# Splitting the gated activations and dividing the attention rows on VectorE, out of a buffer in SBUF

## What is computed

```python
# attention: B, H, S, D = 2, 8, 768, 64; n_sink = 4, window = 128
scores = (q @ k.T) / sqrt(D)
keep = (pos_k < n_sink) | ((0 <= pos_q - pos_k) & (pos_q - pos_k < window))
a = softmax(where(keep, scores, -1e9))          # divided by (sum + 1e-9)
x = (a @ v), heads side by side                 # 1536 tokens x 512
# block 1: 512 -> 2048 -> 512
h = x @ w_in
x = (h * sigmoid(1.702 * h)) @ w_out
# block 2: 512 -> 1536 -> 512
out = (sigmoid(x @ w_gate) * (x @ w_val)) @ w_out2
```

## Time and profile before

| | |
|---|---|
| three executions | 715.40, 715.57, 716.10 us, median 715.57 us |
| the profiled one | 715.4 us, of which the span from first to last instruction is 713.6 us |
| mean granted clock of PE | 0.997 |
| opening stage | 0 to about 87 us |
| chunk 0, 1, 2 | to about 301.6, 521.9 and 711 us |

### The profile page before, as it was taken

How to read it: one execution, slowest core, us unless ns; L and a number is a source line. 1 busy time by engine, 2 the same in 40 slices (tenths; PEclk the granted TensorE clock), 3 DMA queues, 4 the chain that set the end, 5 groups by cost and what they waited for, 6 DMA issues and landing times.

```text
span 713.6 us, 10667 instructions
## 1 busy us (share of the span) xinstructions
PE 687.4 (96%) x3632; PEld 562.0 (79%) x3632; DVE 278.1 (39%) x820; ACT 397.4 (56%) x855; POOL 354.7 (50%) x419
## 2 busy tenths in 40 slices
PE   6777999999999999999999999999999999999998
PEld 5556788888788888788888788888878888788886
DVE  6888434344444333343443433333232222311112
ACT  4787466667665666466676666565444444433321
POOL 2574245555455545266565655464335445544530
PEclk9999999999999999999999999999999999999999
DMA  6322332343433223143325323311132233233001
GB/s 199 137 75 75 114 113 100 101 144 126 141 116 108 89 73 104 60 148 129 99 98 177 125 82 134 119 60 36 60 141 90 91 126 138 103 110 114 0 1 59
DMA packets 23798, 73.41 MB, mean 103 GB/s; under 512 B 3616, under 2 KB 3616, under 8 KB 23744
## 3 DMA queue, kind: packets, MB, share of 16 engines
q1 hardware_dynamic: 23744, 72.73, 30.9%
HBM read 69.57 MB, written 3.15 MB: 102 GB/s over the span
## 4 chain that ended last, share of the span: by engine, by line
PE 88%; ACT 4%; DVE 3%; issue 2%; SPq 1%; DMA 0%; ACTq 0%; DVEq 0%
PE ps L781 22%; PE ps L782 21%; PE ps L783 21%; PE ps L847 5%; PE ps L848 5%; PE ps L849 5%; PE ps L768 1%; PE ps L766 1%; PE ps L767 1%; PE ps L751 1%; PE ps L738 1%; PE ps L752 1%; PE ps L739 1%; ACT probs L434 1%; DVE probs_n L605 1%
## 5 line engine op out<-in xcount | busy, mean ns | idle before, releaser
L379 POOL TENSOR_TENSOR w_lo<-w_raw,w_hi 128x256 fp32r<-128x256 f32 (+1 forms) x336 | 277.4, 857 | 270.7 <-ACT w_hi L428 270.7
L781 PE MATMUL ps<-x_hi,w_hi 128*128 128x512 f32 x480 | 195.6, 407 | 1.2 <-issue 0.9
L782 PE MATMUL ps<-x_lo,w_hi 128*128 128x512 f32 x480 | 188.2, 392 | 0.0
L783 PE MATMUL ps<-x_hi,w_lo 128*128 128x512 f32 x480 | 187.6, 391 | 0.0
L428 ACT ACTIVATE w_hi<-w_raw 128x1024 fp32r<-128x1024 f32 (+1 forms) x84 | 104.3, 1242 | 42.5 <-PE ps L849 25.9
L621 DVE SCALAR_TENSOR_TENSOR ps<-squashed,ps 128x512 f32<-128x512 f32 x84 | 58.2, 692 | 151.2 <-PE ps L783 88.5
L452 ACT ACTIVATE g_hi<-ps 128x512 fp32r<-128x512 f32 x84 | 50.1, 597 | 110.9 <-DVE ps L621 110.9
L783 PEld LDWEIGHTS ps<-x_hi,w_lo 128*128 128x128 f32 x480 | 90.2, 188 | 20.0
L781 PEld LDWEIGHTS ps<-x_hi,w_hi 128*128 128x128 f32 x480 | 90.2, 188 | 15.8 <-issue 1.7
L782 PEld LDWEIGHTS ps<-x_lo,w_hi 128*128 128x128 f32 x480 | 90.6, 189 | 12.8
L626 DVE TENSOR_TENSOR g_lo<-ps,g_hi 128x512 fp32r<-128x512 f32 x84 | 58.0, 691 | 49.5 <-ACT g_hi L452 49.3
(11 more groups left out here) (75 smaller groups left out, 1006.3 us busy)
## 6 DMA issues: line engine op xcount, KB each, us to landing
w_raw<-in_w SPq DMA_DIRECT2D x36, 768.0 KB, 4.3
w_raw<-in_w SPq DMA_DIRECT2D x48, 512.0 KB, 3.3
q_raw<-in_q_t SPq DMA_DIRECT2D x48, 128.0 KB, 3.7
k_raw<-in_k_t SPq DMA_DIRECT2D x48, 128.0 KB, 3.6
v_raw<-in_v_t SPq DMA_DIRECT2D x12, 256.0 KB, 3.7
out_x<-out_sb SPq DMA_DIRECT2D x12, 256.0 KB, 2.2
v_sink_raw<-in_v_sink SPq DMA_DIRECT2D x2, 160.0 KB, 2.9
k_sink_raw<-in_k_sink SPq DMA_DIRECT2D x4, 8.0 KB, 2.2
```

The costliest lines, as they stand in the source:

```text
L379: pool.tensor_tensor(w_lo[:, slot, at:at + part], w_raw[:, slot, at:at + part], w_hi[:, slot, at:at + part].bitcast(F32), ALU.subtract).th ...
L781: pe.matmul(ps[:, bank, :], hi, act_hi, start=first, stop=False)
L782: pe.matmul(ps[:, bank, :], hi, act_lo, start=False, stop=False)
L783: return pe.matmul(ps[:, bank, :], lo, act_hi, start=False, stop=last)
```

## The change

`normalise` of the later units goes from ACT to DVE, right behind `invert`. `gate` writes a new SBUF buffer `gated` and no longer its PSUM bank. `g_high` is taken off ACT; a DVE function `split_gated` makes both parts from `gated`, a copy and a subtraction, and it stands in the same quantum as `gate`, ahead of the attention's instructions of that quantum. PE waits for the banks on `gate_done` in place of `g_ready`; only `down1` and `down2` still wait on `g_ready`. The semaphore `inverted` is dropped, `softmax_steps` counts two a unit. In the opening stage the first `hidden` waits on `masked` in place of `normalised`.

```diff
+        gated = sb("gated", [P, 2, CH])
...
-            def normalise(u):
-                act.wait_ge(inverted, u + 1)
-
-                act.wait_ge(transposed, u - 2)
...
-            def g_high(step):
-                r = step % PER_CHUNK
-                act.wait_ge(gate_done, step + 1)
-
-                wait_step_over(act, step - 2)
-                act.activation(g_hi[:, step % 2, :], ps[:, gated_bank(r), :], ACT.Copy).then_inc(g_hi_done, 1)
...
             def gate(step):
+                r, slot = step % PER_CHUNK, step % 2
                 dve.wait_ge(squash_done, step + 1)
                 dve.wait_ge(hidden_done, step + 1)
-                bank = gated_bank(step % PER_CHUNK)
-                dve.scalar_tensor_tensor(ps[:, bank, :], squashed[:, step % 2, :], 1.0, ps[:, bank, :], ALU.add, ALU.mult).then_inc(gate_done, 1)
-
-            def g_low(step):
+                bank = H_BANKS[r % 2] if r < F1 else VALUE_BANK
+                dve.scalar_tensor_tensor(gated[:, slot, :], squashed[:, slot, :], 1.0, ps[:, bank, :], ALU.add, ALU.mult).then_inc(gate_done, 1)
+
+            def split_gated(step):
                 slot = step % 2
+                dve.wait_ge(gate_done, step + 1)
+
+                wait_step_over(dve, step - 2)
+                dve.tensor_copy(g_hi[:, slot, :], gated[:, slot, :]).then_inc(g_hi_done, 1)
                 dve.wait_ge(g_hi_done, step + 1)
-                dve.tensor_tensor(g_lo[:, slot, :], ps[:, gated_bank(step % PER_CHUNK), :], g_hi[:, slot, :].bitcast(F32),
-                                  ALU.subtract).then_inc(g_ready, 1)
+                dve.tensor_tensor(g_lo[:, slot, :], gated[:, slot, :], g_hi[:, slot, :].bitcast(F32), ALU.subtract).then_inc(g_ready, 1)
...
                     if off == OFF_NORMALISE and n < CHUNK_UNITS:
                         guard(u)
                         invert(u)
+                        normalise(u)
...
                         elif LAST_UP < r < PER_CHUNK - 1:
                             if j == 2 * KT:
                                 gate(step + 1)
-                            if j == 2 * KT + 2:
-                                g_low(step + 1)
+                                split_gated(step + 1)
...
                     if r == LAST_UP:
                         gate(step + 1)
-                        g_low(step + 1)
+                        split_gated(step + 1)
...
-                    wait_from(pe, g_ready, step if r == 0 else step - 1)
+                    wait_from(pe, gate_done, step if r == 0 else step - 1)
...
-                    pe.wait_ge(g_ready, step - 1)
+                    pe.wait_ge(gate_done, step - 1)
...
             def value(step, k):
                 if k == 0:
-                    pe.wait_ge(g_ready, step)
+                    pe.wait_ge(gate_done, step)
...
-                        pe.wait_ge(normalised, early.units)
+                        pe.wait_ge(masked, early.units)
```

More of the change, by code:

```diff
@@ L198, in build @@
         softmax_steps = sem("softmax_steps")
-        inverted = sem("inverted")
         normalised = sem("normalised")
@@ L242, in wait_step_over @@
                     eng.wait_ge(step_done, (PER_CHUNK - 2) * c + r + (1 if r < LAST_UP else 0))
-        def gated_bank(r):
-            return H_BANKS[r % 2] if r < F1 else VALUE_BANK
         def columns_of(step):
@@ L511, in _ @@
             squash(0)
-            g_high(0)
             def attention_at(c, q):
@@ L525, in attention_at @@
                         x_high((u - W_LAG) // GROUP)
-                    if off == OFF_TRANSPOSE and n < CHUNK_UNITS:
-                        normalise(u)
                     if off == OFF_PT and 0 <= n - T_LAG < CHUNK_UNITS:
@@ L540, in _ @@
                             squash(step + 1)
[L541 to L545, removed]
                         if r == PER_CHUNK - 1 and j == quanta_of(c, r) - 1:
@@ L548, in _ @@
                         attention_at(c, first_quantum(c, r) + j)
-                    if r == LAST_UP:
-                        g_high(step + 1)
                 copy_even(c, 2)
@@ L591, in invert @@
             def invert(u):
[L592 to L596, removed]
+                dve.wait_ge(softmax_steps, 2 * u + 1)
+                dve.reciprocal(inverse[:, u % 2:u % 2 + 1], guarded[:, u % 2:u % 2 + 1]).then_inc(softmax_steps, 1)
             def normalise(u):
-                dve.wait_ge(inverted, u + 1)
+                g, h = u // GROUP % 2, u % GROUP
+                dve.wait_ge(softmax_steps, 2 * u + 2)
                 wait_from(dve, transposed, u - 2)
-                g, h = u // GROUP % 2, u % GROUP
                 dve.tensor_scalar(probs_sink[:, g, h * NS:h * NS + NS], probs[:, u % 3, 2 * P:KC],
@@ L675, in _ @@
             gate(0)
-            g_low(0)
+            split_gated(0)
             def attention_at(c, q):
@@ L704, in _ @@
                                 gate(step + 1)
-                            if j == KT + 3:
-                                g_low(step + 1)
+                                split_gated(step + 1)
                         elif LAST_UP < r < PER_CHUNK - 1:
```

## The result

The change costs 4 us. Median of nine executions 720.79 us (718.82 to 724.22), nine of the kernel before beside them 716.94 us; ratio of the means 1.0063, 95% interval 1.0045 to 1.0082, so it is slower by 0.6%, clear of the noise. On the 715.57 us of the forecast that is 720.1, where 719.6 was predicted. The profiled execution took 719.18 us, its span 717.4 against 713.6 us, with the same mean granted clock of 0.997.

A forecast was written before the change was run, and what follows sets the result against it. PE, busy 96% of the span, was taken as the bound, so only its few waits count. The terms -1.2 + 1.2 + 1.0 + 1.8 + 0.5 + 0.7 = +4.0 took 715.57 to 719.6 us, range 715.6 to 721.8.

The forecast's parts named there:

- (d): Step 24: POOL's keys and queries hold DVE's copy and subtraction, PE's score waits for `pt_low`; 0.9, twice: +1.8 us.
- (b): Step 15, g needed at once: POOL holds the split; +0.25 twice, +0.7 in chunk 2, sum +1.2 us.
- (c): Step 23: the split now comes ahead of `pt_low`, POOL idle; +0.5, twice: +1.0 us.
- (e): Step 22: mask 1.95 us later, reaching PE by way of `pt_low`; 0 to 0.6, at 0.25, twice: +0.5 us.
- (f): Step 16: POOL's four weight parts now lie on DVE's split; 0 to 0.7, at 0.35, twice: +0.7 us.
- (a): Chunk ends: PE's banks are free at the product, so the wait of 0.60 us goes, twice: -1.2 us.
- The first: Rival: the subtraction with two SBUF sources doesn't wait for POOL; +0.8 us, 716.4; chance 0.20.
- The second: Rival: ACT, rid of 212 instructions, hands over sooner and hides every queue on DVE; -1.6 us, 714.0; chance 0.12.
- The third: Rival: the division on DVE meets POOL at five more places a chunk, at 0.25 each; 722.1 us; chance 0.12.

The follow-up runs named there:

- e4: The kernel before with only the product written to `gated` and PE waiting on `gate_done`; copy on ACT, subtraction at its old place: 717.21 us, ratio 0.9993.
- e6: The kernel before with the subtraction for step 27 one quantum earlier, no buffer: 715.66 us, ratio 0.9979.
- e3: The changed kernel with the weights' low parts filled with zeros by a POOL memset in place of a subtraction: 719.45 us, one run.
- e8: The changed kernel with both halves of the split two quanta later, where the subtraction had stood: 718.32 us, ratio 1.0012.
- e9: The changed kernel with POOL waiting by a semaphore for `pt_low` before the keys' and queries' low parts: 722.21 us, ratio 1.0073.
- e10: The kernel before with only the division (`normalise`) moved from ACT to DVE: 717.18 us, ratio 1.0000.
- e1: The changed kernel with product, copy and subtraction in the PSUM bank, PE waiting for banks on `g_ready`: 718.53 us, ratio 1.0017.
- e2: The changed kernel with the division (`normalise`) back on ACT: 726.27 us, ratio 1.0115.

## Why the prediction was right, step by step

The forecast was +4.0 and the trace has +3.8, by the mechanism that was named. That the sum came so near is partly luck: (d) was 0.62 too high, (b), (c) and (e) together 0.69 too low. The upper end of the forecast by the bounds of (d), (e) and (f) was added up wrong, too: 2.4, 1.2 and 1.4 give 721.6 us and not 721.0; the measurement lies below either.

**(a)** was right in size (0.60 and a restart of 0.08). e4 and e6 show the cause: the wait on the bank.

**(b)** was 0.3 short, +0.32, +0.33 and +0.82 where +0.25, +0.25 and +0.7 stood. The way was as told: the copy held once in chunk 0, copy and subtraction both in chunk 2. Every hand-over between POOL and DVE took a little more than was put down; the subtraction of chunk 2 was held for 0.69 us where 0.6 had been counted.

**(c)** was short by the restart: +0.55 and +0.57 of wait where 0.5 stood. No contention is in it (e3 keeps it, e8 removes it).

**(d)** was mis-sized. For chunk 0 the 0.6 to 1.2 held, with the upper end: the queries got their turn ahead of DVE's subtraction, and PE lost 1.11 and the restart. But the term was doubled, by the sentence that chunk 1 repeats the places of chunk 0. The last group of units of chunk 1 has no successor whose keys must be split, and POOL is idle at 493. The rows that would have told were in the trace of before:

```profile
489.39 0.70 DVE L621 SCALAR_TENSOR_TENSOR ps<-squashed,ps 128x512 f32<-128x512 f32 x1 [1.44 <-PE ps L783]
...
494.02 3.94 POOL L379 TENSOR_TENSOR w_lo<-w_raw,w_hi 128x384 fp32r<-128x384 f32 x4 [5.75 <-ACT w_hi L428]
```

The product for the same step in chunk 1 stands in the middle of 5.75 us in which POOL does nothing. e9 shows that keys and queries were the cause in chunk 0.

**(e)** was right in size, +0.5 against +0.65, and wrong in its way: not `pt_low` and a score, but the mask and a transpose. PE's transpose for a unit waits for the mask of the next unit, and the mask stood behind the held copy of 1.20 us and the subtraction. The mask was named there, 1.95 us late by the estimate; who waits for it was not followed.

**(f)** was the middle of 0 and 0.7 and came out at 0.32 and 0.33. e10 and e3 take it apart: both have -0.17 there, ACT's relief, so POOL's weights on the split make +0.5.

**The rivals.** The first fails at the earlier trace rows and its answer above: two sources wait. (e1's +0.93 is near the +0.8 that it gave, but by another sum, with the slower copy in it.) The second named a true gain, ACT's relief, but it is 0.6 us (-0.17 and -0.14, twice), and it does not reach step 23. The third is refuted by e10 and by the table of places. The Trainium skill, SBUF - State Buffer, section Who interferes with whom, says that an instruction with two SBUF inputs contends with a GpSimd instruction that reads SBUF; the traces agree (1.67 us against 0.69).

## What to carry to other kernels

When an intermediate moves from PSUM to SBUF on VectorE, look at what GpSimd runs at the moments when the next product waits for that result; here the faster copy (0.43 against 0.69 us) lost to waits of up to 1 us. Count a term once for every place where the trace shows its conditions, not once for every round of a loop: the last round often lacks the work for the next. And a wait on a buffer may be had away by moving the instruction that frees it, as e6 did with one line, before a buffer is added.

## What the runs showed of the hardware that was not expected

**The clock in the opening stage.** In that stage PE is often idle, and its granted clock falls to half for a few microseconds: once in the profiled executions of the kernel before and of the change, two to six times in the others, at places that differ from one to the next. e2's profile, windows of 1 us (length, busy us of PE, PEld, DVE, ACT, POOL, then the granted clock, DMA share, GB/s):

```profile
64.00:65.00 1.00, 0.50 (x3) 0.07 (x1) 0.70 (x5) 1.00 (x3) 0.02 (x1) 1.00 0.42 131
65.00:66.00 1.00, 0.00 (x0) 0.00 (x0) 0.49 (x2) 1.00 (x5) 1.00 (x1) 1.00 0.00 0
66.00:67.00 1.00, 0.41 (x5) 0.41 (x6) 1.00 (x7) 0.26 (x2) 0.92 (x2) 1.00 0.00 0
67.00:68.00 1.00, 1.00 (x10) 1.00 (x9) 0.95 (x4) 0.91 (x4) 0.92 (x2) 0.59 0.09 25
68.00:69.00 1.00, 1.00 (x5) 0.70 (x5) 0.82 (x5) 0.91 (x3) 0.55 (x1) 0.50 0.02 6
```

PE did 0.91 us of work in 3 us, and then ran at 0.50, 1.2 GHz of 2.4, from about 67.2 on. The same came once after the opening stage, in e2 behind the wait of 1.99 us at 284.18 shown above, and cost about 1.5 us of lag. At 95 us the kernels lag the one before by 0.0 (the change) to 6.1 us (e2), though their instructions up to there are nearly the same. The kernel before alone, in one set of thirty, ran in 715.5 to 720.4 us, its mean granted clock 0.997 to 0.985. That is why the kernels were compared from 95 us on. That the spread of the executions that were not profiled has this origin is inferred from their clocks and not seen.

**A memset holds a copy, not a subtraction.** In e3, at step 16 of chunk 1:

```profile
418.15 1.78 POOL L376 MEMSET w_lo<- 128x384 f32 x4 [7.34 <-ACT w_hi L424]
...
418.50 0.71 DVE L594 CAST g_hi<-gated 128x512 fp32r<-128x512 f32 x1
419.24 0.69 DVE L596 TENSOR_TENSOR g_lo<-gated,g_hi 128x512 fp32r<-128x512 f32 x1
```

The copy took 0.28 us longer beside memsets, the subtraction with two sources nothing; step 16 of chunk 0 reads the same (0.71 and 0.69). The Trainium skill, SBUF - State Buffer, section Who interferes with whom, says that a GpSimd instruction that only writes SBUF is no hindrance to one with two SBUF inputs, while copies can take both ports; this case agrees with both.
